# Finishing the preceding step's down tiles first, in a fused two-layer feed-forward kernel

## The chip, the cores and the metric

The kernel runs on one core of a Trainium2 chip. The metric is the device time of one execution in microseconds. TensorE (PE) does the matmuls, ScalarE (ACT) the activations and copies, VectorE (DVE) the elementwise work, SyncE (SP) issues the transfers, GpSimd (POOL) helps at the start.

## The reference

Three stages over 8192 tokens of 192 values, all float32:

```python
x = attn(x, weight_gen)                 # softmax over 7 taps, a causal window of 7 tokens, 8 heads
g = x @ w_gate                          # layer 1, 192 -> 1536
x = (g * sigmoid(g)) * (x @ w_val) @ w_out
h = x @ w_in                            # layer 2, 192 -> 2048
x = (h * clip(h + 3, 0, 6) / 6) @ w_out2
```

## The kernel before, in words

**Blocks and periods.** The tokens are cut into BLOCKS = 16 blocks of 512 columns. Period i (0 to 16) does layer 1 of block i and layer 2 of block i-1. Layer 1 has N1 = 12 tiles of 128 hidden units, layer 2 has N2 = 16; tiles are numbered n = 0 to 11 and N1 + 0 to N1 + 15. Periods 2 to 14 are a loop, the others are written out.

**Precision.** Each float32 operand is split into a rounded high part (hi) and a remainder (lo), and a product is taken as hi x hi, hi x lo (of the weights) and hi x lo (of the data). ACT makes the high parts (L438 for the hidden values), DVE the remainders (L672).

**Tiles.** An up product gives a hidden tile, a down product adds it to the layer's sum. D = 192 = 128 + 64, and the 64 left over (the tail) is packed. On PE everything works on half of the array's rows: LOW is the first 64 partitions, HIGH the last 64, and an instruction in one half can run beside one in the other. An up bank of PSUM is begun by one half and finished by the other; `s_halves` keeps them apart. The sums of a layer are the accumulator pair `acc1` or `acc2`; `s_down_half` separates the halves there.

**Steps.** PE's order is written out by hand. `gated_step` handles one tile of layer 1 (gate and value: 18 half-instructions) and one down product (10). `plain_step` handles two tiles of layer 2 (18) and two down products (20). A down product lags by LAG = 4 tiles, and `hid_hi` and `hid_lo` are rings of RING = 4. In both steps the order is: begin the up banks, begin the down products, finish the up banks, finish the down products. Plain step j handles tiles N1+2j and N1+2j+1 and takes down N1+2j-4 and N1+2j-3.

**Other engines.** Per tile, ACT does `bend` (Silu L429 in layer 1, Relu L431 in layer 2) and then `round_hi` of the tile before; DVE does `tile_product` (L664 or L667), `between(i, n, 0)`, `tile_lo` of the tile before (L672), `between(i, n, 1)`. `bend` of a tile waits for `tile_lo` two tiles back, since there are two hidden buffers; `round_hi` waits until the ring's place is free (`s_down`). `between` hands out the other work one piece at a time: the 18 operations of the next block's convolution (k = 2n + slot), `fold_output` (L704) at n = 10, `input2_lo` (L692) at n = 9, `sum_tail` (L698) at n = N1+3, and `input1_lo` (L679, L686) at n = N1+7 and N1+8. ACT has `take_sum2` at n = 4, `take_rows` at n = N1, `take_sum1` at n = N1+3, `input1_hi` (L450, L453) at n = N1+7.

**Transposes.** `transpose_output(i-2)` (L980, L985) stands between the gated and the plain steps and writes to `acc2`. `transpose_input(i+1)` (L961, L967) stands after plain step j = 3 and writes to `acc1`. Both are twelve small instructions.

**Waits of a down product.** `down_ready` (L813) waits for `s_hid_lo` of its tile and, at the first tile of a layer, for the accumulators to be free: for layer 2 that is `s_out_rows`, the copy of the output rows. `up_ready` waits for `s_hidden`, the products of all tiles up to two steps back.

Of the kernel before, what the change touches and what calls it, by code (L numbers as in the profile page):

```python
# [35 lines left out]
P = 128  # L36
# [3 lines left out]
LAG = 4  # L40
WARM_SLOTS = 66
# [3 lines left out]
def swiglu_hardswish_kernel(nc, x, taps_in, w_gate, w_val, w1_out, w2_in, w2_out, out):  # L45
# [54 lines left out]
    with ExitStack() as ctx:  # L100
# [128 lines left out]
        def input_banks(b):  # L229


            return acc_pair[2 if isinstance(b, int) and b == 1 else 1]
# [46 lines left out]
        def _(sp):  # L279
            def load_piece(q):  # L280
# [6 lines left out]
                elif kind == "tail":  # L287
                    for half in range(2):
                        dst = buf[half * TAIL:(half + 1) * TAIL, 0:CW // y]
                        if y == 1:  # L290
                            src = (w_val, w_gate)[half][P:D, col:col + CW]
                        else:
                            dst = dst.rearrange("r (j c) -> r j c", c=P)
                            src = w[P:D, col:col + CW].rearrange("r (j b c) -> r j b c", b=2, c=P)[:, :, 1 - half, :]
                        sp.dma_start(dst, src).then_inc(s_stage[q % STAGES], 16)
# [106 lines left out]
        def _(act):  # L402
# [44 lines left out]
            def input1_hi(b):  # L447
                banks = input_banks(b)
                act.wait_ge(s_in_cols, b + 1)
                nc.scalar.copy(by_half(inp[1]["hi"][:, :]), main_cols(banks)).then_inc(s_in1_hi, 1)  # L450
                for par in range(2):
                    for half in halves:
                        last = nc.scalar.copy(by_parity_half(inp[1]["tail_hi"][half, :])[:, :, par, :, :],  # L453
                                              tail_cols(banks, halves[par]))
                last.then_inc(s_in1_hi, 1)
# [29 lines left out]
            def period(i):  # L485
# [11 lines left out]
                for n in tiles:  # L497
# [14 lines left out]
                    if n == (N1 + 3 if fixed(i, BLOCKS) else N1) and has_out:  # L512
                        take_rows(i - 2)
                    if n == N1 + 3 and not fixed(i, BLOCKS):
                        take_sum1(i)
                    if n == N1 + 7 and has_next:
                        input1_hi(i + 1)
                if fixed(i, 0):
                    round_hi(i, N1 - 1)
                    input1_hi(1)  # L520
                    take_sum1(0)
# [10 lines left out]
            input1_hi(0)  # L532
            periods(act, period)
# [8 lines left out]
        def _(dve):  # L542
# [132 lines left out]
            def input1_lo(b, part):  # L675
# [6 lines left out]
                for par in range(2):  # L682
                    for half in halves:
                        hi, lo = (by_parity_half(inp[1][name][half, :])[:, :, par, :, :]
                                  for name in ("tail_hi", "tail_lo"))
                        last = nc.vector.tensor_tensor(lo, tail_cols(banks, halves[par]), as_f32(hi), ALU.subtract)  # L686
                last.then_inc(s_in1_lo, 1)
# [21 lines left out]
            def between(i, n, slot):  # L709

                has_next = not (fixed(i, BLOCKS - 1) or fixed(i, BLOCKS))
                k = 2 * n + slot - (HALF + 1 if fixed(i, 0) else 0)
                if k < -HALF:
# [9 lines left out]
                elif n == N1 - 2 and slot == 0 and not (fixed(i, 0) or fixed(i, 1) or fixed(i, BLOCKS)):  # L723
                    fold_output(i - 2)
                elif n == N1 - 3 and not fixed(i, 0):
                    input2_lo(i - 1, slot)
                elif n == N1 + 3 and slot == 1 and not fixed(i, BLOCKS):
                    sum_tail(i)
                elif n in (N1 + 7, N1 + 8) and slot == 1 and has_next:
                    input1_lo(i + 1, n - N1 - 7)  # L730

            def period(i):
# [13 lines left out]
                if fixed(i, 0):  # L746
                    tile_lo(i, N1 - 1)
                    input1_lo(1, 0)
                    input1_lo(1, 1)
                    sum_tail(0)  # L750
# [16 lines left out]
            input1_lo(0, 1)  # L767
            shift_max(rest[PARTS - 2], rest[PARTS - 1])
# [5 lines left out]
        def _(pe):  # L774
# [38 lines left out]
            def down_ready(i, n):  # L813
# [4 lines left out]
                if i == 1 and n == 0:  # L818
                    pe.wait_ge(s_mid, 1)
                if y == 2 and k == 0 and i < BLOCKS:  # L820
                    wait(pe, s_out_rows, i - 1)
# [16 lines left out]
            def operands(at):  # L838
                _, kind, n = steps[at]
                even, odd = up_bank[2 * (n % 2)], up_bank[2 * (n % 2) + 1]  # L840
                if kind == "gated":
                    return 1, (even, n * P), (odd, F1 + n * P), n * P
                return 2, (even, 2 * n * P), (odd, (2 * n + 1) * P), n * P

            def up_halves(at):
                y, (even, even_col), (odd, odd_col), _ = operands(at)
                up_ready(at)
                for product in range(3):
                    up_main(LOW, even, y, even_col, product, first=True)
                    mm = up_main(HIGH, odd, y, odd_col, product, first=True)  # L850
                mm.then_inc(s_halves, 1)

            def up_alone(at):
                up_halves(at)
                up_halves(at + 1)
                for one in (at, at + 1):
                    y, (even, even_col), (odd, odd_col), col = operands(one)
                    pe.wait_ge(s_halves, one + 1)
                    for product in range(3):
                        up_main(HIGH, even, y, even_col, product)  # L860
                        up_main(LOW, odd, y, odd_col, product)
                    for product in range(2):
                        up_tail(HIGH, even, y, col, product)
                        up_tail(LOW, odd, y, col, product)
                    up_tail(HIGH, even, y, col, 2).then_inc(s_first, 1)
                    up_tail(LOW, odd, y, col, 2).then_inc(s_val if y == 1 else s_first, 1)

            def gated_step(i, n, di, d):
                at = number[i, "gated", n]
                y, (gate, gate_col), (val, val_col), col = operands(at)  # L870
                down_steps[0] += 1
                up_halves(at)
                wait(pe, s_down, tile_no(di, d))
                down_ready(di, d)
# [4 lines left out]
                down_main(LOW, d, 2).then_inc(s_down_half, 1)  # L879
                pe.wait_ge(s_halves, at + 1)  # L880
                up_main(HIGH, gate, y, gate_col, 0)
                up_main(LOW, val, y, val_col, 0)
                up_main(HIGH, gate, y, gate_col, 1)
                up_main(LOW, val, y, val_col, 1)
                up_main(HIGH, gate, y, gate_col, 2)
                up_main(LOW, val, y, val_col, 2)
                up_tail(HIGH, gate, y, col, 0)
                up_tail(LOW, val, y, col, 0)
                up_tail(HIGH, gate, y, col, 1)
                up_tail(LOW, val, y, col, 1)  # L890
                up_tail(HIGH, gate, y, col, 2).then_inc(s_first, 1)
                up_tail(LOW, val, y, col, 2).then_inc(s_val, 1)
                pe.wait_ge(s_down_half, down_steps[0])
                down_main(HIGH, d, 0)
                down_tail(LOW, d, 0)
                down_main(HIGH, d, 1)
                down_tail(LOW, d, 1)
                down_main(HIGH, d, 2).then_inc(s_down, 1)

            def plain_step(i, j, c, d):  # L900
                at = number[i, "plain", j]
                y, (even, even_col), (odd, odd_col), col = operands(at)
                down_steps[0] += 1
                up_halves(at)
                wait(pe, s_down, tile_no(i, c))
                down_ready(i, c)
                down_main(LOW, c, 0)
                down_tail(HIGH, c, 0)
                down_main(LOW, c, 1)
                down_tail(HIGH, c, 1)  # L910
                down_main(LOW, c, 2)
                down_ready(i, d)
                down_tail(HIGH, d, 0)
                down_main(LOW, d, 0)
                down_tail(HIGH, d, 1)
                down_main(LOW, d, 1)
                pe.wait_ge(s_halves, at + 1)
                up_main(HIGH, even, y, even_col, 0)
                down_main(LOW, d, 2).then_inc(s_down_half, 1)
                up_main(HIGH, even, y, even_col, 1)  # L920
                up_main(LOW, odd, y, odd_col, 0)
                up_main(HIGH, even, y, even_col, 2)
                up_main(LOW, odd, y, odd_col, 1)
                up_tail(HIGH, even, y, col, 0)
                up_main(LOW, odd, y, odd_col, 2)
                up_tail(HIGH, even, y, col, 1)
                up_tail(LOW, odd, y, col, 0)
                up_tail(HIGH, even, y, col, 2).then_inc(s_first, 1)
                up_tail(LOW, odd, y, col, 1)
                pe.wait_ge(s_down_half, down_steps[0])  # L930
                down_main(HIGH, c, 0)
                up_tail(LOW, odd, y, col, 2).then_inc(s_first, 1)
                down_main(HIGH, c, 1)
                down_tail(LOW, c, 0)
                down_main(HIGH, c, 2)
                down_tail(LOW, c, 1).then_inc(s_down, 1)
                down_main(HIGH, d, 0)
                down_tail(LOW, d, 0)
# [115 lines left out]
```

## Time and profile before

| | us |
|---|---|
| median of 3 runs | 1271.58 (1271.38 to 1272.57) |
| the profiled execution | 1271.35 |
| its span, first to last instruction | 1269.5 |
| PE busy | 1220.7 |
| DVE busy | 881.0 |
| ACT busy | 650.9 |

The profile is of one execution. A timeline row gives the start, the time, the engine and line, the operation, what it writes and reads, and the count of merged instructions; a bracket holds the engine's idle time before it and what ended it. A merged row (x2) covers both instructions from the first's start to the last's end. PE is the matmuls, PEld the weight loads, which overlap them. In the mean PE is busy in 96% of the span, and the chain that ended last runs through it for 70%.

### The profile page before, as it was taken

To read this page: it belongs to the slowest core of one execution; us is meant where nothing else is said; L and a number is where in the kernel's file an instruction comes from. 1 tells how busy PE (TensorE), PEld (TensorE's weight loads), DVE (VectorE), ACT (ScalarE), POOL (GpSimd) and SP (SyncE) were. 2 spreads that over 40 slices of the span, in tenths; PEclk is the share of its full clock that TensorE was granted. 3 is DMA by queue.
4 is the path that set the end of the run, shared out by engine and by line. 5 is a ranking of instruction groups with operands and counts; after the bars stand their busy time and mean duration, and the time that the engine had idled before them with its cause. 6 is when DMAs were issued, how large, how long until landed. Compare 5 with 4: busy or idle time off the path is not lost.

```text
span 1269.5 us, 26488 instructions
## 1 busy us (share of the span) xinstructions
PE 1220.7 (96%) x10696; PEld 1032.1 (81%) x10696; DVE 881.0 (69%) x1353; ACT 650.9 (51%) x1178; POOL 57.6 (5%) x43
## 2 busy tenths in 40 slices
PE   5779999999999999999999999999999999999998
PEld 4557888888898888888888888888889888888876
DVE  7688676676867768686776867667686766864554
ACT  1554654546455453645546464554645545364554
POOL 6441100000000000000000000000000000000000
PEclk9899999999999999999999999999999999999999
DMA  5330001001010100101000010100101010000000
GB/s 163 87 112 23 11 1 44 2 1 44 1 45 1 39 7 1 45 1 44 1 22 24 1 44 2 44 1 7 39 2 44 1 44 2 1 13 1 14 13 14
DMA packets 11766, 32.00 MB, mean 25 GB/s; under 512 B 1048, under 2 KB 5784, under 8 KB 11544
## 3 DMA queue, kind: packets, MB, share of 16 engines
q1 hardware_dynamic: 11672, 30.53, 7.4%
q8 instruction: 85, 1.39, 0.5%
q14 instruction: 9, 0.07, 0.0%
HBM read 24.24 MB, written 6.29 MB: 24 GB/s over the span
## 4 chain that ended last, share of the span: by engine, by line
PE 70%; DVE 13%; ACT 11%; issue 3%; DMA 1%; POOL 0%; ACTq 0%; SPq 0%; POOLq 0%
PE up_bank L787 27%; PE acc L802 16%; PE up_bank L793 14%; PE acc L809 11%; DVE hid_lo L672 6%; DVE hidden L667 5%; ACT hidden L431 5%; DVE in_tail_lo L686 2%; ACT hid_hi L438 1%; PE up_bank L1024 1%; ACT in_tail_hi L453 1%; DMA stage<-in_moe_w_gate_dram 1%; DMA stage<-in_moe_w_val_dram 1%; ACT in_hi L450 1%; ACT swapped L461 1%
## 5 line engine op out<-in xcount | busy, mean ns | idle before, releaser
L787 PE MATMUL up_bank<-in_hi,up_hi 64*128 64x512 f32 x1280 | 350.7, 395 | 18.0 <-DVE hidden L664 12.3
L809 PE MATMUL acc<-hid_hi,dn_tail 64*128 64x512 f32 x872 | 342.4, 393 | 11.6 <-DVE hid_lo L672 10.7
L787 PE MATMUL up_bank<-in_hi,up_lo 64*128 64x512 f32 x1280 | 346.2, 388 | 0.0
L787 PE MATMUL up_bank<-in_lo,up_hi 64*128 64x512 f32 x1280 | 345.9, 388 | 0.0
L802 PE MATMUL acc<-hid_hi,dn_hi 64*128 64x512 f32 x872 | 342.3, 393 | 0.0
L802 PE MATMUL acc<-hid_lo,dn_hi 64*128 64x512 f32 x872 | 337.4, 387 | 0.0
L802 PE MATMUL acc<-hid_hi,dn_lo 64*128 64x512 f32 x872 | 337.3, 387 | 0.0
L809 PE MATMUL acc<-hid_lo,dn_tail 64*128 64x512 f32 x872 | 337.3, 387 | 0.0
L667 DVE SCALAR_TENSOR_TENSOR hidden<-hidden,up_bank 128x512 f32<-128x512 f32 x256 | 176.1, 688 | 209.7 <-ACT hidden L431 208.5
L672 DVE TENSOR_TENSOR hid_lo<-hidden,hid_hi 128x512 fp32r<-128x512 f32 x448 | 313.0, 699 | 1.0
L431 ACT ACTIVATE hidden<-up_bank,half_col 128x512 f32<-128x512 f32 x256 | 176.4, 690 | 242.0 <-DVE hid_lo L672 129.7
L429 ACT ACTIVATE hidden<-up_bank 128x512 f32<-128x512 f32 x192 | 114.9, 598 | 333.2 <-PE up_bank L793 290.8
L438 ACT CAST hid_hi<-hidden 128x512 fp32r<-128x512 f32 x448 | 273.5, 610 | 1.1 <-DVE hidden L667 0.8
L787 PEld LDWEIGHTS up_bank<-in_hi,up_hi 64*128 64x128 f32 x1280 | 198.6, 185 | 44.2 <-DVE hidden L664 18.1
L664 DVE TENSOR_TENSOR hidden<-hidden,up_bank 128x512 f32<-128x512 f32 x192 | 132.0, 687 | 127.3 <-ACT hidden L429 116.0
L787 PEld LDWEIGHTS up_bank<-in_lo,up_hi 64*128 64x128 f32 x1280 | 198.6, 185 | 20.3
L787 PEld LDWEIGHTS up_bank<-in_hi,up_lo 64*128 64x128 f32 x1280 | 198.8, 185 | 19.6
L809 PEld LDWEIGHTS acc<-hid_hi,dn_tail 64*128 64x128 f32 x872 | 160.5, 184 | 41.6 <-DVE hid_lo L672 30.6
L802 PEld LDWEIGHTS acc<-hid_hi,dn_hi 64*128 64x128 f32 x872 | 160.5, 184 | 13.4 <-issue 0.4
L802 PEld LDWEIGHTS acc<-hid_hi,dn_lo 64*128 64x128 f32 x872 | 160.7, 184 | 12.9
L802 PEld LDWEIGHTS acc<-hid_lo,dn_hi 64*128 64x128 f32 x872 | 160.6, 184 | 13.0
L809 PEld LDWEIGHTS acc<-hid_lo,dn_tail 64*128 64x128 f32 x872 | 160.7, 184 | 9.4
(87 smaller groups left out, 1400.1 us busy)
## 6 DMA issues: line engine op xcount, KB each, us to landing
window<-in_x_dram SPq DMA_DIRECT2D x14, 960.0 KB
out_dram<-out_rows SPq DMA_DIRECT2D x16, 384.0 KB, 2.3
stage<-in_moe_w_out_dram SPq DMA_DIRECT2D x7, 384.0 KB, 3.5
window<-in_x_dram SPq DMA_DIRECT2D x4, 472.5 KB
taps<-in_weight_gen_dram SPq DMA_DIRECT2D x1, 1568.0 KB, 13.0
stage<-in_moe_w_in_dram SPq DMA_DIRECT2D x4, 256.0 KB, 2.7
stage<-in_moe_w_gate_dram SPq DMA_DIRECT2D x3, 256.0 KB, 2.7
stage<-in_moe_w_val_dram SPq DMA_DIRECT2D x3, 256.0 KB, 8.3
```

The costliest lines, as they stand in the source:

```text
L429: nc.scalar.activation(buf, up_bank[2 * (n % 2)][:, :], ACT.Silu).then_inc(s_bent, 1)
L431: nc.scalar.activation(buf, up_bank[n % 4][:, :], ACT.Relu, bias=half_col[:, 0:1], scale=1.0 / 6.0).then_inc(s_bent, 1)
L438: nc.scalar.copy(hid_hi[:, n % RING, :], hidden[:, n % 2, :]).then_inc(s_hid_hi, 1)
L450: nc.scalar.copy(by_half(inp[1]["hi"][:, :]), main_cols(banks)).then_inc(s_in1_hi, 1)
L664: nc.vector.tensor_tensor(buf, buf, up_bank[2 * (n % 2) + 1][:, :], ALU.mult).then_inc(s_hidden, 1)
L667: nc.vector.scalar_tensor_tensor(out=buf, in0=buf, scalar=1.0, in1=up_bank[n % 4][:, :], op0=ALU.min, op1=ALU.mult).then_inc(s_hidden, 1)
L672: nc.vector.tensor_tensor(hid_lo[:, n % RING, :], hidden[:, n % 2, :], as_f32(hid_hi[:, n % RING, :]), ALU.subtract).then_inc(s_hid_lo, 1)
L686: last = nc.vector.tensor_tensor(lo, tail_cols(banks, halves[par]), as_f32(hi), ALU.subtract)
L787: return nc.tensor.matmul(dst[:, :], w[lane[half], col:col + P], a[lane[half], :], start=first and product == 0, stop=False)
L793: return nc.tensor.matmul(dst[:, :], w[lane[half], col:col + P], a[lane[half], :], start=False, stop=product == 2)
L802: return nc.tensor.matmul(acc[y][0], w[lane[half], k, :], a[lane[half], n % RING, :], start=half == LOW and product == 0 and k == 0, stop= ...
L809: return nc.tensor.matmul(acc[y][1], dn_tail[y][lane[half], k, :], a[lane[half], n % RING, :], start=half == HIGH and product == 0 and k == 0,
```

## The change

A step now first finishes the down products that the step before began, and begins its own as its last act. In layer 2 the HIGH half runs one instruction ahead: the first up product of step j+1 is issued at the end of step j (`up_first_high`). The steps are written out for each kind of neighbour (`gated_after_plain`, `plain_after_gated`, openings, `finish_downs`). LAG and RING stay at 4, and each product is computed as before.

Moved besides: `transpose_output` to after gated step 7 with `fold_output` at n = 6 (the later convolution operations shift by one place) and `take_rows` at n = 9; `transpose_input` to after gated step 11, now into `acc2` for all blocks but the first; `input1_hi` to n = N1, N1+1 and N1+2 in three pieces; `input1_lo` to n = N1+2, N1+3, N1+4, slot 1, in three pieces; `input2_lo` to n = 10; `take_sum1` to n = N1+4, `sum_tail` to n = N1+5. The first down product of layer 2 now waits for `s_in1_lo` at 2i+4, which is the last piece of `input1_lo(i+1)`; in period 15 it waits for `s_out_rows`.

```diff
         def input_banks(b):
-            return acc_pair[2 if isinstance(b, int) and b == 1 else 1]
+            return acc_pair[1 if isinstance(b, int) and b == 0 else 2]
...
                 k = 2 * n + slot - (HALF + 1 if fixed(i, 0) else 0)
+                if has_out and (n, slot) == (FOLD_AT, 0):
+                    fold_output(i - 2)
+                    return
+                if has_out and n >= FOLD_AT:
+                    k -= 1
...
-                elif n == N1 - 3 and not fixed(i, 0):
+                elif n == N1 - 2 and not fixed(i, 0):
                     input2_lo(i - 1, slot)
-                elif n == N1 + 3 and slot == 1 and not fixed(i, BLOCKS):
+                elif n in (N1 + 2, N1 + 3, N1 + 4) and slot == 1 and has_next:
+                    input1_lo(i + 1, n - N1 - 2)
+                elif n == N1 + 5 and slot == 1 and not fixed(i, BLOCKS):
                     sum_tail(i)
-                elif n in (N1 + 7, N1 + 8) and slot == 1 and has_next:
-                    input1_lo(i + 1, n - N1 - 7)
...
-                if y == 2 and k == 0 and i < BLOCKS:
-                    wait(pe, s_out_rows, i - 1)
+                if y == 2 and k == 0 and i < BLOCKS - 1:
+                    pe.wait_ge(s_in1_lo, 2 * i + 4)
+                elif y == 2 and k == 0 and i == BLOCKS - 1:
+                    pe.wait_ge(s_out_rows, i - 1)
...
+            def gated_step(i, n, p, di, d):
+                at = number[i, "gated", n]
+                up_begin(at)
+                may_finish_downs()
+                down_tail(LOW, p, 0)
+                down_main(HIGH, p, 0)
+                down_tail(LOW, p, 1)
+                down_main(HIGH, p, 1)
+                pe.wait_ge(s_halves, at + 1)
+                low_up(at, 0)
+                down_main(HIGH, p, 2).then_inc(s_down, 1)
+                low_up(at, 1)
+                high_up(at, 0)
...
+                low_up(at, 5)
+                high_up(at, 4)
+                may_begin_down(di, d)
+                down_main(LOW, d, 0)
+                high_up(at, 5)
+                down_main(LOW, d, 1)
+                down_tail(HIGH, d, 0)
+                down_main(LOW, d, 2)
+                down_tail(HIGH, d, 1).then_inc(s_down_half, 1)
...
+            def begin_two_downs(i, j, c, d, last_up):
+                may_begin_down(i, c)
+                down_main(LOW, c, 0)
+                last_up()
+                down_main(LOW, c, 1)
+                down_tail(HIGH, c, 0)
+                down_main(LOW, c, 2)
+                down_tail(HIGH, c, 1)
+                down_ready(i, d)
...
+                down_main(LOW, d, 2).then_inc(s_down_half, 1)
+                if j + 1 < N2 // 2:
+                    up_first_high(number[i, "plain", j + 1])
+                elif i + 1 < BLOCKS:
+                    up_first_high(number[i + 1, "gated", 0])
...
+            def plain_step(i, j, p, q, c, d):
+                at = number[i, "plain", j]
+                up_begin(at, begun=True)
+                may_finish_downs()
+                down_main(HIGH, p, 0)
...
+                low_up(at, 5)
+                high_up(at, 4)
+                begin_two_downs(i, j, c, d, lambda: high_up(at, 5))
...
             def transpose_input(b):
                 pe.wait_ge(s_conv_rows, b + 1)
                 banks = input_banks(b)
-                if b != 1:
-                    wait(pe, s_mid, b)
+                if b > 2:
+                    pe.wait_ge(s_out_rows, b - 2)
...
+                    if n == ROWS_AFTER and i >= 2:
+                        transpose_output(i - 2)
+                if i + 1 < BLOCKS:
+                    transpose_input(i + 1)
+                for j in range(N2 // 2):
+                    c = N1 + 2 * j - LAG
+                    if j == 0:
+                        plain_after_gated(i, c - 1, c, c + 1)
+                    else:
+                        plain_step(i, j, c - 2, c - 1, c, c + 1)
```

## Rows read from the trace of the kernel before

**Rows 1.** The page's head: busy time and share of the span.

```profile
PE 1220.7 (96%) x10696; PEld 1032.1 (81%) x10696; DVE 881.0 (69%) x1353; ACT 650.9 (51%) x1178; POOL 57.6 (5%) x43
```

**Rows 2.** Timeline of PE: start us, us, engine, line, operation; two gated steps.

```profile
620.90 0.61 PE L787 MATMUL up_bank<-in_hi,up_hi 64*128 64x512 f32 x2
621.12 0.61 PE L787 MATMUL up_bank<-in_hi,up_lo 64*128 64x512 f32 x2
...
624.07 0.61 PE L787 MATMUL up_bank<-in_hi,up_hi 64*128 64x512 f32 x2
```

**Rows 3.** Timeline of PE at the output transposes of two periods and an input group.

```profile
655.81 0.44 PE L980 MATMUL acc<-ident,out_main 64*128 64x64 f32 x5
...
674.05 0.44 PE L961 MATMUL acc<-ident,conv_main 64*128 64x64 f32 x5
...
674.74 0.57 PE L787 MATMUL up_bank<-in_hi,up_lo 64*128 64x512 f32 x2
...
731.02 0.28 PE L980 MATMUL acc<-ident,out_main 64*128 64x64 f32 x2
```

**Rows 4.** Waits (total us, times, longest): whole run, then 656 to 731 us.

```profile
PEld acc L809 <- DVE hid_lo L672: 30.6, 45, 1.5
...
PEld acc L809 <- DVE hid_lo L672: 2.0, 3, 0.9
```

**Rows 5.** Timeline around one such wait.

```profile
670.21 0.68 DVE L672 TENSOR_TENSOR hid_lo<-hidden,hid_hi 128x512 fp32r<-128x512 f32 x1
...
670.95 0.49 PE L809 MATMUL acc<-hid_hi,dn_tail 64*128 64x512 f32 x1 [0.21 <-DVE hid_lo L672]
...
671.28 0.39 PE L809 MATMUL acc<-hid_lo,dn_tail 64*128 64x512 f32 x1
```

**Rows 6.** Timelines of ACT and DVE in a calm plain step.

```profile
687.69 0.69 ACT L431 ACTIVATE hidden<-up_bank,half_col 128x512 f32<-128x512 f32 x1 [0.93 <-PE up_bank L793]
...
689.82 0.69 ACT L431 ACTIVATE hidden<-up_bank,half_col 128x512 f32<-128x512 f32 x1 [0.93 <-DVE hid_lo L672]
...
688.41 0.69 DVE L667 SCALAR_TENSOR_TENSOR hidden<-hidden,up_bank 128x512 f32<-128x512 f32 x1 [0.84 <-ACT hidden L431]
689.02 0.68 DVE L672 TENSOR_TENSOR hid_lo<-hidden,hid_hi 128x512 fp32r<-128x512 f32 x1
```

**Rows 7.** Timeline of PE: a matmul that waits for the one before it.

```profile
92.42 0.39 PE L952 MATMUL acc<-hid_lo,dn_tail 128*128 128x512 f32 x1
...
92.86 0.19 PEld L948 LDWEIGHTS acc<-hid_hi,dn_hi 128*128 128x128 f32 x1 [0.48 <-PE acc L952]
...
93.20 0.40 PE L949 MATMUL acc<-hid_hi,dn_lo 128*128 128x512 f32 x1
```

**Rows 8.** Timeline: the last up matmul of a tile, and ACT on its bank.

```profile
651.95 0.39 PE L793 MATMUL up_bank<-in_tail_lo,up_tail_hi 64*128 64x512 f32 x2
...
652.37 0.60 ACT L429 ACTIVATE hidden<-up_bank 128x512 f32<-128x512 f32 x1 [2.07 <-PE up_bank L793]
```

**Rows 9.** Timeline of DVE, 676 to 681 us: the first two tail operations of the split.

```profile
679.68 0.68 DVE L672 TENSOR_TENSOR hid_lo<-hidden,hid_hi 128x512 fp32r<-128x512 f32 x1
680.29 0.84 DVE L686 TENSOR_TENSOR in_tail_lo<-acc,in_tail_hi 64x256 fp32r<-64x256 f32 x2
```

**Rows 10.** PE in stretches (us, busy, count, granted clock, DMA, GB/s), then its timeline.

```profile
51.30:54.10 2.80, 0.01 (x2) 1.00 0.62 178
...
55.30:58.70 3.40, 3.40 (x18) 0.50 0.13 39
...
62.80:64.40 1.60, 0.00 (x0) 1.00 0.71 219
64.50:67.90 3.40, 3.40 (x28) 1.00 0.24 78
...
55.80 1.05 PE L787 MATMUL up_bank<-in_hi,up_lo 64*128 64x512 f32 x2
56.22 1.05 PE L787 MATMUL up_bank<-in_lo,up_hi 64*128 64x512 f32 x2
```

More of the change, by code:

```diff
@@ L681, in input1_lo @@
                     return
[L682 to L687, printed above, removed]
+                par = part - 1
+                for half in halves:
+                    hi, lo = (by_parity_half(inp[1][name][half, :])[:, :, par, :, :]
+                              for name in ("tail_hi", "tail_lo"))
+                    last = nc.vector.tensor_tensor(lo, tail_cols(banks, halves[par]), as_f32(hi), ALU.subtract)
+                if par == 1:
+                    last.then_inc(s_in1_lo, 1)
             def input2_lo(b, part):
@@ L839, in operands @@
                 _, kind, n = steps[at]
-                even, odd = up_bank[2 * (n % 2)], up_bank[2 * (n % 2) + 1]
+                first, second = up_bank[2 * (n % 2)], up_bank[2 * (n % 2) + 1]
                 if kind == "gated":
[L842 to L846, printed above, removed]
-                up_ready(at)
[L848 to L851, printed above, removed]
+                    return 1, (first, n * P), (second, F1 + n * P), n * P
@@ new lines, in operands, with up_begin @@
+                return 2, (second, (2 * n + 1) * P), (first, 2 * n * P), n * P
+            def up_begin(at, begun=False):
+                y, (x, x_col), (z, z_col), _ = operands(at)
+                if not begun:
+                    up_ready(at)
+                    up_main(LOW, x, y, x_col, 0, first=True)
+                    up_main(HIGH, z, y, z_col, 0, first=True)
+                    up_main(LOW, x, y, x_col, 1)
+                    up_main(HIGH, z, y, z_col, 1)
+                    up_main(LOW, x, y, x_col, 2)
+                    up_main(HIGH, z, y, z_col, 2).then_inc(s_halves, 1)
+                else:
+                    up_main(LOW, x, y, x_col, 0, first=True)
+                    up_main(HIGH, z, y, z_col, 1)
+                    up_main(LOW, x, y, x_col, 1)
+                    up_main(HIGH, z, y, z_col, 2)
+                    up_main(LOW, x, y, x_col, 2).then_inc(s_halves, 1)
@@ L853, in up_alone @@
             def up_alone(at):
-                up_halves(at)
-                up_halves(at + 1)
+                up_begin(at)
+                up_begin(at + 1)
                 for one in (at, at + 1):
-                    y, (even, even_col), (odd, odd_col), col = operands(one)
                     pe.wait_ge(s_halves, one + 1)
[L859 to L866, printed above, removed]
@@ L868, in gated_step, with may_finish_downs @@
-            def gated_step(i, n, di, d):
-                at = number[i, "gated", n]
-                y, (gate, gate_col), (val, val_col), col = operands(at)
-                down_steps[0] += 1
-                up_halves(at)
-                wait(pe, s_down, tile_no(di, d))
-                down_ready(di, d)
+                    for k in range(6):
+                        low_up(one, k)
+                        high_up(one, k)
+            def may_finish_downs():
+                pe.wait_ge(s_down_half, down_steps[0])
@@ L943, in down_alone, with finish_downs @@
+            def finish_downs(*tiles):
+                may_finish_downs()
+                for n in tiles:
+                    down_tail(LOW, n, 0)
+                    down_main(HIGH, n, 0)
+                    down_tail(LOW, n, 1)
+                    down_main(HIGH, n, 1)
+                    down_main(HIGH, n, 2).then_inc(s_down, 1)
             def down_alone(i, n):
@@ new lines, in last_period @@
+            def last_period(i):
+                finish_downs(TILES - LAG - 2, TILES - LAG - 1)
+                for n in range(TILES - LAG, TILES):
+                    down_alone(i - 1, n)
+                up_alone(number[i, "plain", 0])
+                transpose_output(i - 2)
+                for j in range(2, N2 // 2):
+                    c = N1 + 2 * j - LAG
+                    if j == 2:
+                        plain_opening(i, j, c, c + 1)
+                    else:
+                        plain_step(i, j, c - 2, c - 1, c, c + 1)
+                finish_downs(TILES - LAG - 2, TILES - LAG - 1)
+                for n in range(TILES - LAG, TILES):
+                    down_alone(i, n)
@@ L1027, in _ @@
             transpose_input(0)
-            for i in range(BLOCKS + 1):
+            first_period()
+            for i in range(1, BLOCKS):
                 period(i)
+            last_period(BLOCKS)
             transpose_output(BLOCKS - 1)
```

271 lines of the change are left out of this document (173 added, 98 removed).

## The prediction

> **What bounds the kernel now.** First the page's head: PE is busy 1220.7 of 1269.5 us, DVE 881.0, ACT about half of it [rows 1]. So TensorE is the bound, but a busy engine says nothing of whether it could go faster; for that I read its timeline. An instruction here works on one half of the array's rows (lane LOW or HIGH), and two run side by side. In both lanes starts follow each other at 0.2266 us; I call this a slot. A gated step has 28 half-instructions, 14 slots, and one step starts 3.17 us after the last, which is 14 x 0.2266 [rows 2]. So a gated step has no hole at all. A plain step (two tiles, 38 halves) would be 19 slots, 4.31 us.
>
> Next I ask what a period costs over its slots. 12 gated and 8 plain steps are 12 x 14 + 8 x 19 = 320 slots, 72.50 us. The output transposes of two neighbouring periods start at 655.81 and 731.02, 75.21 apart [rows 3]. 2.71 us are over. The group of the input starts at 674.05 and the second up product behind it at 674.74, where without transposes it would be 0.23 behind [rows 3]: 0.46 us, and as much for the output group, 0.92 together. The remaining 1.79 us per period are waits, and the list of waits names them: weight loads of the down product at L809 for DVE's hid_lo, 45 in the run, 3 in this period, 1.5 us at most [rows 4]. One of them shows their shape: LOW and HIGH stop, the load starts with its matmul at 670.95, 0.06 us after hid_lo ends at 670.89, and the matmul behind it comes 0.33 us after the first instead of 0.23, so a restart costs 0.11 more [rows 5]. They all lie in layer 2, in the steps where DVE and ACT have extra work (the sum of layer 1, the split of the next input). Periods 1 to 14 hold 42 of them and period 15 has 2; at 1.6 to 1.8 us a period and 0.9 in the last I put them at 25.2 us in all. The 45th, in period 16, is about 1.4 us.
>
> **The down product begun last.** Nothing is added: a gated step is still 28 halves, a plain one 38, in strict alternation of the lanes. The first down product of a plain step starts in slot 14 instead of 4, its second in slot 17 instead of about 6, so hid_lo may come about 10 slots, 2.4 us, later. The largest wait seen is 1.5 us [rows 4]. All 45 waits fall within that margin: -25.2 -1.4 = -26.6 us. What is late next? The up bank of step j+1 is asked for at the end of step j and needs the product of the second tile of step j-1. From a calm step: first Relu 0, its product +0.72, hid_lo +1.33, next first Relu +4.31, a step later [rows 6]; the second Relu of a step comes at +2.13 and its product ends at +3.54, and PE asks at about +5.0. So 1.4 us are spare. The ring of four is tighter: hid_hi of a step's first tile now has to wait for a down product that finishes in slot 5 of the next step. That step starts at -0.42 - 12 slots + 4.31 = +1.17, its slot 5 at +2.08, seen 0.42 later at +2.5; ACT is there at +2.7. 0.2 us spare, no cost.
>
> Waits inside PE: what a later matmul may see of an earlier one is 0.44 us from start to weight load, with 0.11 more to the matmul [rows 7], 0.55 in all. The new gated step asks for its halves 3 slots (0.68 us) after they start, 0.57 at least where the lanes stand half a slot apart. The weight load normally starts one slot ahead of the matmul, at 0.45. I cost it at nothing; from both sides it is 0 to 0.1 us in some 170 gated steps.
>
> **Transposes and the input work moved.** The two transpose groups stay at 0.46 us. The output group now follows gated step 7 and needs DVE's fold, put at tile 6 in place of one convolution step; the fold takes 0.84 us like its neighbours, and step 7 ends 1 us later than that. The convolution ends at tile 9, the input group comes after tile 11: spare. SP's window load hangs on the convolution and its store on the rows copied out at tile 9 instead of 12: neither is later, and no DMA is added. ACT's and DVE's pieces of the input split, one per tile, fit in the time in which each waits for the other [rows 6].
>
> But the input transposes now land in the second accumulator pair, where layer 2 sums. So down_ready has a new wait: the first down product of layer 2 waits until the whole of input i+1 is split (s_in1_lo at 2i+4). That product is tile c of plain step j=2 (c = N1+2j-4). And the last piece of the split is given out by DVE at n = N1+4, slot 1: behind the product of tile N1+4 and hid_lo of N1+3. Tile N1+4 is the first tile of this same step j=2, whose up product ends just before. PE can't be served before DVE has gone through that tile. The chain, from the start of the last up matmul of N1+4:
> - PE to ACT 0.42 (matmul 651.95, Silu 652.37) [rows 8]
> - Relu to DVE's product 0.72, product to hid_lo 0.61 [rows 6]
> - hid_lo to the tail split 0.61, two of its 64x256 operations 0.84 [rows 9]
> - end on DVE to weight load 0.06 [rows 5]
>
> Sum 3.26. Without the wait the matmul would start 0.23 after that up matmul; with it 0.11 after the late load. Hole: 3.26 + 0.11 - 0.23 = 3.14 us. No slack elsewhere shortens it, since the producer's input comes from PE itself two instructions earlier. Behind the waiting load in PE's queue stand the last up product of the second tile, both down products and the next step's first up; ACT waits for the first of these. ACT and DVE have caught up by then, so the later steps are calm. Condition: has_next, i = 1 to 14. 14 x 3.14 = +44.0 us. Period 15 waits for out_rows there, long done.
>
> **Edges.** Six places wait at once for what has just been issued (the two openings of the down products, the plain opening, three times finish_downs): 0.44 + 0.11 - 0.23 = 0.32 each [rows 7], and three unpaired slots of 0.23: 2.6 us. Those of the first period stand beside ACT and DVE, which set its pace. I take +2.0; bounds 0 and 2.6.
>
> **The clock.** 1271.6 - 26.6 + 44.0 + 2.0 = 1291 would be all if TensorE kept its clock. In each hole it stands idle for 2.9 us (3.26 less the 0.39 of the matmul running). The trace has a hole of 2.8 us in the first period, and 1.2 us behind its end the granted clock is 0.50 (1.2 GHz) for 3.4 us, starts 0.42 us apart instead of 0.23; behind a hole of 1.6 us it stays 1.00 (2.4 GHz) [rows 10]. At half clock 3.4 us hold 8 slots instead of 15: 7 x 0.2266 = 1.6 us lost. The new hole is of the larger kind. The fall in the trace came with a delay, so where a hole lies decides whether it comes; I take 10 of 14, +16 us, with 0 and 14 (+22) as bounds. Sum: 1307.
>
> The Trainium skill has a rule here (page "TensorE: Matmul & The Clock Gate", section on HAM oscillation in real kernels): where every round of a loop has a wait long enough to re-throttle, the transition is paid in every round and not once. By that rule all 14 would pay, which gives 1291 + 22 = 1313; the trace agrees as far as one hole of 2.8 us can show it.
>
> **Rivals.**
> 1. The hole as computed, the clock holds in most of them: 1291 (1286 to 1297). For it: two holes of 1.6 cost no clock, and one event is thin evidence. Against: 2.9 is above the 2.8 that did.
> 2. More waits than one: the halves in gated steps are asked for too early. It decides once lanes stand more than half a slot apart, as they do behind the transposes. 0.1 us in each of 170 steps is +17: about 1324. Against: a late lane corrects itself, because only the leading lane waits.
> 3. Faster: the new wait is met in time and only the gain is left, 1271.6 - 26.6 + 2.0 = 1247. This decides if the split of the input ends 3.2 us earlier than DVE's order has it, one tile pair. Against it stands the order written out in between(), which I followed tile by tile; for it, only an error of mine in that.
> That the change doesn't do what it says would be that the old waits stay as well: 1307 + 26.6. For that hid_lo would have to come 2.4 us later than it was wanted, and the longest wait is 1.5 [rows 4]; its chance is within rival 2's.
>
> **How the numbers follow.** The sum is made against the profiled execution, 1271.35 us (span 1269.5), which is 0.2 from the median of 1271.58. Forecast 1307 with chance 0.68, own range 1298 to 1316; rival 1 0.19; rival 2 0.08; rival 3 0.05. Range 1286 to 1318: it leaves out rival 3, most of rival 2 and the thin ends. 0.2% is 2.5 us, about what a measurement of this kernel tells from no change. Slower: the first three, 0.94; faster 0.05; 0.01 for a meeting in the middle.
>
> **What would show it.** In the profile after: no PE wait for hid_lo at L809 in layer 2; instead one wait per period for in_tail_lo, 14 in all, each near 3.1 us, PE's largest; the distance of output transposes about 76.6 us, or some 78 where the clock fell; a granted clock below 1.00 in stretches of 3.4 us behind the holes, mean about 0.98. Wrong would be: no such wait, a second family of waits, or a clock row that stays 1.00.

## The result and the profile after

The changed kernel takes 1317.47 us (1316.96 to 1317.64, 4 runs), the one before 1272.07 us (1271.38 to 1272.98). The ratio is 1.0356 with a 95% interval of 1.0338 to 1.0374: 3.6% slower. The forecast was 1307 us with a range of 1286 to 1318.

The head of the profile after, to be read against [rows 1]: the same number of matmuls, a span longer by 46 us, and PE busy for a smaller share of it.

```profile
span 1315.7 us, 26501 instructions
PE 1233.1 (94%) x10696; PEld 1076.9 (82%) x10696; DVE 880.4 (67%) x1353; ACT 652.6 (50%) x1178; POOL 57.1 (4%) x43
```

PE's list of waits after (total us, times, longest). The line that answers to [rows 4], for hid_lo, is gone; the first line is new.

```profile
PE acc L821 <- DVE in_tail_lo L698: 43.3, 14, 3.1
PE up_bank L806 <- DVE hidden L676: 13.8, 10, 2.7
PE up_bank L1203 <- ACT up_hi L410: 12.2, 1, 12.2
PE up_bank L806 <- DVE in_tail_lo L698: 4.4, 1, 4.4
```

14 waits of up to 3.1 us, one in each of periods 1 to 14. The other three lines are the start and the first two periods, as in the kernel before. The timeline of one such wait, ACT, DVE and PE sorted by start, with lines left out:

```profile
612.65 0.39 PE L812 MATMUL up_bank<-in_tail_lo,up_tail_hi 64*128 64x512 f32 x1
...
613.07 0.69 ACT L433 ACTIVATE hidden<-up_bank,half_col 128x512 f32<-128x512 f32 x1 [1.06 <-PE up_bank L812]
...
613.79 0.69 DVE L679 SCALAR_TENSOR_TENSOR hidden<-hidden,up_bank 128x512 f32<-128x512 f32 x1 [0.21 <-ACT hidden L433]
...
614.40 0.69 DVE L684 TENSOR_TENSOR hid_lo<-hidden,hid_hi 128x512 fp32r<-128x512 f32 x1
...
615.12 0.87 DVE L698 TENSOR_TENSOR in_tail_lo<-acc,in_tail_hi 64x256 fp32r<-64x256 f32 x2
...
616.13 0.48 PE L821 MATMUL acc<-hid_hi,dn_hi 64*128 64x512 f32 x1 [3.09 <-DVE in_tail_lo L698]
616.13 0.54 PE L812 MATMUL up_bank<-in_tail_lo,up_tail_hi 64*128 64x512 f32 x1
```

It is the chain of the forecast, link by link: the last up matmul of tile N1+4, its Relu, its product, hid_lo of the tile before, the last piece of the input's split, and only then the first down product of layer 2. From 612.65 to 616.13 are 3.48 us. The last row shows what is queued behind the wait: the last up product of the second tile.

PE in stretches around it (stretch, us, busy, count, granted clock, DMA share, GB/s):

```profile
591.00:613.00 22.00, 22.00 (x204) 1.00 0.18 63
613.10:616.10 3.00, 0.00 (x0) 1.00 0.00 0
616.40:619.80 3.40, 3.40 (x18) 0.51 0.02 5
619.90:666.00 46.10, 46.10 (x410) 1.00 0.00 1
```

Behind the hole the granted clock is 0.51, that is 1.2 GHz, for 3.4 us. The trace shows such a stretch at the end of every one of the 14 holes; it begins 0.1 us before the end of the first and 0.7 us behind the end of the last. The mean clock of the run is 0.978 instead of 0.996. The rows that answer to [rows 3], the output transposes of two neighbouring periods:

```profile
588.16 0.40 PE L1136 MATMUL acc<-ident,out_main 64*128 64x64 f32 x8
...
666.61 0.41 PE L1136 MATMUL acc<-ident,out_main 64*128 64x64 f32 x8
```

78.45 us lie between them, 75.21 before. 3.24 more in 14 periods are 45.4 us, which is the whole loss.

### The profile page after: what moved, and what is told of

Same layout as the page of the kernel before. It is cut to its first block, busy times and chain, and to the rows that moved or that the text cites. A ratio compares the mean times of both kernels' runs of the same rounds, so it can differ in the third digit from the quotient of the medians.

```text
span 1315.7 us, 26501 instructions
## 1 busy us (share of the span) xinstructions
PE 1233.1 (94%) x10696; PEld 1076.9 (82%) x10696; DVE 880.4 (67%) x1353; ACT 652.6 (50%) x1178; POOL 57.1 (4%) x43
## 4 chain that ended last, share of the span: by engine, by line
PE 89%; DVE 6%; ACT 2%; DMA 1%; issue 1%; POOL 0%; SPq 0%; ACTq 0%; DVEq 0%; POOLq 0%
PE up_bank L806 33%; PE acc L821 23%; PE up_bank L812 16%; PE acc L828 15%; DVE hid_lo L684 1%; DVE in_tail_lo L698 1%; ACT hidden L433 1%; DVE hidden L679 1%; DMA window<-in_x_dram 1%; DMA stage<-in_moe_w_val_dram 1%; DVE prod_even L571 1%; PE acc L1104 0%; DVE prod_odd L571 0%; PE acc L1117 0%; DVE sum_even L575 0%
## 5 line engine op out<-in xcount | busy, mean ns | idle before, releaser
L806 PE MATMUL up_bank<-in_hi,up_hi 64*128 64x512 f32 x1280 | 360.6, 400 | 19.4 <-DVE hidden L676 13.8
L806 PE MATMUL up_bank<-in_hi,up_lo 64*128 64x512 f32 x1280 | 355.3, 393 | 0.0
L806 PE MATMUL up_bank<-in_lo,up_hi 64*128 64x512 f32 x1280 | 354.3, 392 | 0.0
L828 PE MATMUL acc<-hid_lo,dn_tail 64*128 64x512 f32 x872 | 343.7, 394 | 0.0
L821 PE MATMUL acc<-hid_lo,dn_hi 64*128 64x512 f32 x872 | 343.5, 394 | 0.0
L821 PE MATMUL acc<-hid_hi,dn_lo 64*128 64x512 f32 x872 | 343.3, 394 | 0.0
L806 PEld LDWEIGHTS up_bank<-in_hi,up_hi 64*128 64x128 f32 x1280 | 203.1, 188 | 44.0 <-DVE hidden L676 19.7
L812 PE MATMUL up_bank<-in_tail_lo,up_tail_hi 64*128 64x512 f32 x640 | 203.7, 391 | 0.0
L812 PE MATMUL up_bank<-in_tail_hi,up_tail_hi 64*128 64x512 f32 x640 | 199.0, 387 | 0.0
L812 PE MATMUL up_bank<-in_tail_hi,up_tail_lo 64*128 64x512 f32 x640 | 198.8, 387 | 0.0
```

The source lines that it names most:

```text
L806: return nc.tensor.matmul(dst[:, :], w[lane[half], col:col + P], a[lane[half], :], start=first and product == 0, stop=False)
L812: return nc.tensor.matmul(dst[:, :], w[lane[half], col:col + P], a[lane[half], :], start=False, stop=product == 2)
L821: return nc.tensor.matmul(acc[y][0], w[lane[half], k, :], a[lane[half], n % RING, :], start=half == LOW and product == 0 and k == 0, stop= ...
L828: return nc.tensor.matmul(acc[y][1], dn_tail[y][lane[half], k, :], a[lane[half], n % RING, :], start=half == HIGH and product == 0 and k == 0,
```

## The experiments

The rivals were: (A) the wait for the input's split and the clock behind it are the whole loss; (B) the new order of the steps costs something itself; (C) the clock falls, or not, for another reason. All times are medians. A ratio is to the kernel before, run on the same chip.

**The input work put back (e1_input_later).** All else of the change stays.

```diff
-            return acc_pair[1 if isinstance(b, int) and b == 0 else 2]
+            return acc_pair[2 if isinstance(b, int) and b == 1 else 1]
-                    if n == N1 and has_next:
+                    if n == N1 + 7 and has_next:
                         input1_hi(i + 1)
-                elif n in (N1 + 2, N1 + 3, N1 + 4) and slot == 1 and has_next:
-                    input1_lo(i + 1, n - N1 - 2)
+                elif n in (N1 + 9, N1 + 10, N1 + 11) and slot == 1 and has_next:
+                    input1_lo(i + 1, n - N1 - 9)
-                if y == 2 and k == 0 and i < BLOCKS - 1:
-                    pe.wait_ge(s_in1_lo, 2 * i + 4)
...
+                if y == 2 and k == 0 and i < BLOCKS:
+                    wait(pe, s_out_rows, i - 1)
...
+                    if j == 3 and i + 1 < BLOCKS:
+                        transpose_input(i + 1)
```

> The changed kernel with one part undone: the input transposes stand after plain step 3 again and write to acc1, ACT's pieces of the split come at tiles N1+7 to N1+9 and DVE's at N1+9 to N1+11, and the first down product of layer 2 waits for the copied output rows as in the kernel before. The new order of the down products, the upper half ahead and the moved output work stay. Theory (all of the loss is the wait for the input split and the clock behind it, 3.4 + 1.65 us a period): no wait of PE in layer 2, granted clock 1.00 after the start, 1317.5 - 14 x 5.05 = 1247 us. Rival (the new order of the steps costs something by itself): above 1260 us, with PE waits in gated steps or inside PE. Rival that the old waits for hid_lo stay: about 1272 us.

Measured: 1251.01 us against 1271.81, ratio 0.9836 (0.9819 to 0.9852). The 14 waits are gone, no wait for hid_lo has come in their place, and the clock stays at 1.00 after the first period. So the new order costs nothing that shows here; B falls. 4 us are missing to the 1247 expected: the periods last 73.73 us, 0.28 more than in the next run. The timeline of PE's weight loads shows them idle ahead of the input transposes, for nothing that the profile names:

```profile
590.35 0.36 PEld L1115 LDWEIGHTS acc<-ident,conv_main 64*128 64x128 f32 x8 [0.35 <-issue]
```

There the transposes stand between an up product already begun in one half and the rest of it; whether that is the reason is asked below.

**The split given out two tiles earlier (e4_two_earlier).** The wait stays in PE's program.

```diff
-                    if n == N1 and has_next:
+                    if n == N1 - 1 and has_next and not fixed(i, 0):
                         input1_hi(i + 1)
-                    if n in (N1 + 1, N1 + 2) and has_next:
-                        input1_tail_hi(i + 1, n - N1 - 1)
+                    if n in (N1 - 1, N1) and has_next and not fixed(i, 0):
+                        input1_tail_hi(i + 1, n - N1 + 1)
-                elif n in (N1 + 2, N1 + 3, N1 + 4) and slot == 1 and has_next:
-                    input1_lo(i + 1, n - N1 - 2)
+                elif n in (N1, N1 + 1, N1 + 2) and slot == 1 and has_next:
+                    input1_lo(i + 1, n - N1)
-                if i + 1 < BLOCKS:
-                    transpose_input(i + 1)
...
+                    if n == N1 - 2 and i + 1 < BLOCKS:
+                        transpose_input(i + 1)
```

> The changed kernel with the input transposes after gated step 10 instead of 11, and every piece of the input split on ACT and DVE given out earlier, so that DVE's last piece is at tile N1+2 instead of N1+4. The wait on PE stays, in the same place. Theory: the last piece ends about 1 us before PE asks, no hole, clock 1.00, 1317.5 - 14 x 5.05 = 1247 us, like the kernel with the input work put back. Rival (it isn't the time of the last piece but the sharing of acc2 or the wait itself that costs): stays above 1290 us.

Measured: 1247.07 us, ratio 0.9803 (0.9787 to 0.982). It beats both kernels by changing only when the pieces are given out, and with them the input transposes, one gated step earlier. The output transposes of two periods:

```profile
558.47 0.35 PE L1136 MATMUL acc<-ident,out_main 64*128 64x64 f32 x6
...
631.92 0.29 PE L1136 MATMUL acc<-ident,out_main 64*128 64x64 f32 x4
```

73.45 us, that is 72.50 of slots and 0.95 for the two groups of transposes: no hole is left in a period. Neither the sharing of acc2 nor the wait as such costs anything.

**One tile earlier (e3_one_earlier).** As above, by one tile: DVE's pieces at N1+1 to N1+3, and the input transposes stay after gated step 11.

```diff
-                    if n in (N1 + 1, N1 + 2) and has_next:
-                        input1_tail_hi(i + 1, n - N1 - 1)
+                    if n in (N1, N1 + 1) and has_next:
+                        input1_tail_hi(i + 1, n - N1)
-                elif n in (N1 + 2, N1 + 3, N1 + 4) and slot == 1 and has_next:
-                    input1_lo(i + 1, n - N1 - 2)
+                elif n in (N1 + 1, N1 + 2, N1 + 3) and slot == 1 and has_next:
+                    input1_lo(i + 1, n - N1 - 1)
```

> The changed kernel with ACT's and DVE's pieces of the input split one tile earlier, DVE's last at N1+3. Theory: the piece no longer depends on the first tile of step 2; from the Relu of tile N1+2 it ends at +4.9 us, PE asks at +3.9, so a hole of about 1.2 us instead of 3.4 stays, 14 times. A hole of that size is below the one of 1.6 us behind which the clock stayed in the kernel before, so the clock stays at 1.00: 1317.5 - 14 x (3.4 - 1.2 + 1.65) = 1264 us. Rival (any hole brings the clock down): 1264 + 23 = 1287 us. Rival (the hole isn't set by DVE's order): 1317 us.

Measured: 1265.77 us, ratio 0.9953 (0.9937 to 0.997). The list of waits has the same line with a third of the time, and the clock stays at 1.00:

```profile
PE acc L821 <- DVE in_tail_lo L698: 14.0, 14, 1.0
```

The three places of the last piece in DVE's order give a series: N1+4 is 3.6% slower than before, N1+3 0.5% faster, N1+2 2.0% faster.

**The hole filled (e2_fill).** The pairs compute nothing that is used. Their number, FILLS, is 12.

```diff
+                if j == 2 and i < BLOCKS - 1:
+                    fill(number[i, "plain", j + 1])
                 may_begin_down(i, c)
```

> The changed kernel with 12 pairs of matmuls put ahead of the wait in plain step 2; their results go to the up banks of the next step, which it overwrites. 12 x 0.2266 = 2.7 us of otherwise empty work in a hole of 3.1 us idle. Theory: the hole stays as long as it was, since DVE sets its end, but the granted clock stays at 1.00, which gives back 14 x 1.65 = 23 us: 1294 us. Rival (the clock falls for something else in that step): it falls 14 times as before and the time is 1317 us. Rival (the filling delays the chain): above 1317 us.

Measured: 1295.17 us, ratio 1.0185 (1.0168 to 1.0202). PE's idle time in the hole is down to 0.4 us (list of waits), and the clock stays (stretch behind it, columns as above):

```profile
PE acc L822 <- DVE in_tail_lo L699: 5.3, 14, 0.4
```

```profile
613.00:680.00 67.00, 67.00 (x610) 1.00 0.06 22
```

The distance to the changed kernel is 22.3 us, 1.59 per hole: the price of the clock, separated from that of the hole.

**Half filled (e8_fill4, e10_fill6).** The same with 4 and with 6 pairs.

> The changed kernel with 4 pairs of empty matmuls ahead of the wait instead of 12, so that TensorE is idle for about 2.2 us in each hole, between the 1.7 us that kept the clock and the 2.75 us that didn't. The hole ends where it did. If each such hole costs the clock: 1317 us. If none does: 1294 us, as with 12 pairs. My reading in the prediction (the place of the hole decides): some pay and some don't, 1300 to 1312 us, and stretches of 0.50 in the clock rows behind only part of the 14 holes.

Measured with 4 pairs: 1316.42 us, ratio 1.0352 (1.0331 to 1.0372). 13 of 14 holes cost the clock. The first hole and the second:

```profile
142.30:144.50 2.20, 0.00 (x0) 1.00 0.00 0
144.60:148.00 3.40, 3.40 (x30) 1.00 0.00 0
219.20:221.30 2.10, 0.00 (x0) 1.00 0.00 0
222.00:225.40 3.40, 3.40 (x20) 0.50 0.00 0
```

Both are 2.2 us; the first is followed by 30 matmuls in 3.4 us, the second by 20 in the same time at half clock.

> The changed kernel with 6 pairs of empty matmuls ahead of the wait, idle time in the hole about 1.75 us. With 4 pairs and 2.2 us idle, 13 of 14 holes cost the clock; the holes of 1.6 and 1.77 us in the first period of several runs cost nothing. If size alone decides: the clock stays 1.00, 1294 us. If the place of the hole decides too: some pay, 1297 to 1312 us. If it doesn't matter how long TensorE is idle but only that it waits: 1317 us.

Measured with 6 pairs: 1294.57 us, ratio 1.0186 (1.0157 to 1.0216); no hole costs the clock, with up to 1.8 us idle:

```profile
PE acc L822 <- DVE in_tail_lo L699: 24.3, 14, 1.8
```

So at this place up to 1.8 us cost nothing in 14 of 14 holes, 2.2 us the clock in 13 of 14, 3.1 us in 14 of 14. That size decides alone is not shown: the holes of one run lie alike, and the first period, where PE waits for DVE's products, shows the contrary. In the run with the input work put back it has a hole of 3.17 us behind which the clock stays at 1.00; in the 1247 us run the hole at the same place, 3.10 us, has the clock at 0.50 from 53.5 to 60.3:

```profile
54.29 0.50 PE L806 MATMUL up_bank<-in_hi,up_hi 64*128 64x512 f32 x2 [3.17 <-DVE hidden L676]
51.20:54.20 3.00, 0.00 (x0) 1.00 0.69 181
54.30:57.70 3.40, 3.40 (x28) 1.00 0.15 39
```

```profile
51.60:54.50 2.90, 0.00 (x0) 0.82 0.75 190
54.60:60.20 5.60, 5.60 (x26) 0.50 0.09 24
```

The first three rows (one of the timeline, then two stretches) are of e1_input_later, the other two of e4_two_earlier.

**A longer hole (e5_longer).** DVE's sum of the layer 1 tail is put ahead of the last piece.

```diff
                 elif n in (N1 + 2, N1 + 3, N1 + 4) and slot == 1 and has_next:
+                    if n == N1 + 4:
+                        sum_tail(i)
                     input1_lo(i + 1, n - N1 - 2)
```

> The changed kernel with DVE's sum of layer 1's tail ahead of the last piece of the input split, both at tile N1+4. The sum waits for ACT's copies, which end 2.9 us behind the Relu of that tile, so the last piece ends at about +4.4 instead of +2.9. Theory (DVE's order sets the end of the hole): PE's idle time in it 4.5 instead of 3.1 us, 14 x 1.45 = 20 us more, 1338 us, with the clock falling once behind each hole for 3.4 us. Rival (the chain is bounded by something else, PE's own restart say): 1317 us. Rival (a longer hole costs the clock for longer): up to 1361 us.

Measured: 1345.42 us, ratio 1.058 (1.0559 to 1.0601), 7 us over the expectation. PE's idle time is 4.7 us in each hole, as computed to 0.2; so DVE's order sets the end. The rest is clock: at 8 of the 14 holes it is low for 6.8 us instead of 3.4, which lies between the theory and the rival of a longer loss. One of the 8, and one of the 6:

```profile
543.70:548.30 4.60, 0.00 (x0) 0.93 0.00 0
548.40:551.00 2.60, 2.60 (x12) 0.50 0.00 0
551.00:554.40 3.40, 3.40 (x18) 0.50 0.00 0
```

```profile
625.00:629.60 4.60, 0.00 (x0) 1.00 0.00 0
629.70:633.00 3.30, 3.30 (x16) 0.50 0.02 5
633.00:636.40 3.40, 3.40 (x32) 1.00 0.00 0
```

All 14 holes are 4.7 us long, so the two kinds don't differ in size. In the 8 the clock falls 0.7 to 1.8 us before PE starts again, in the 6 at most 0.6 us before.

**The moves without the new order (e6_old_order).** The steps of the kernel before, with the moves of the 1247 us run.

```diff
             def plain_step(i, j, c, d):
                 at = number[i, "plain", j]
...
                 up_halves(at)
                 wait(pe, s_down, tile_no(i, c))
                 down_ready(i, c)
                 down_main(LOW, c, 0)
...
+                        if n == N1 - 2 and 0 < i < BLOCKS - 1:
+                            transpose_input(i + 1)
```

> The moves alone: transposes, fold, copied rows and input work as in the run with DVE's last piece at tile N1+2 (1247 us), but PE's steps in the order of the kernel before (own down products in the middle of the step, no upper half ahead; the layer 2 tail weights in their old halves). Theory (the new order buys about 2.4 us of margin for hid_lo, the old one has next to none): the first down product of layer 2 is asked for at slot 4 of step 2, 1.3 us before the split of the input is done, a hole of about 1.3 us; the wait for hid_lo behind the sum of layer 1 stays at about 0.6, and some small ones: 72.5 + 0.9 + 1.3 + 0.6 + 0.3 = 75.6 us a period, about 1277 us, clock 1.00. Rival (the margin comes from giving the input work out in small pieces earlier, and the order of the down products doesn't matter): about 1250 us.

Measured: 1275.74 us, ratio 1.0031 (1.0018 to 1.0043). PE waits for both things:

```profile
PEld acc L828 <- DVE hid_lo L684: 10.4, 17, 1.5
...
PE acc L821 <- DVE in_tail_lo L698: 14.9, 14, 1.1
```

With the same moves the new order is worth 1275.74 - 1247.07 = 28.7 us. Of the old 45 waits for hid_lo 17 are left in spite of the old order, so a part of them came from where the extra work stood. With the new order neither wait is left. The rival (the order doesn't matter) falls.

**No upper half ahead (e7_no_slot_ahead).** On the 1247 us run.

```diff
-                if j + 1 < N2 // 2:
-                    up_first_high(number[i, "plain", j + 1])
-                elif i + 1 < BLOCKS:
-                    up_first_high(number[i + 1, "gated", 0])
```

> The run with DVE's last piece at tile N1+2 (1247 us), but without the upper half ahead in layer 2: the first upper up product is issued in its own step again. Theory (a plain step is 38 halves in two lanes of 19 either way, and no wait inside PE comes nearer than 3 slots): 1247 us within 2 us, periods of 73.45 us. Rival (the slot ahead hides a latency between the halves): 0.1 to 0.3 us more in each of some 120 plain steps, 1259 us or more.

Measured: 1246.93 us, ratio 0.9804 (0.9788 to 0.982), the same as with it. This part of the change is worth nothing here.

**No upper half ahead, input work put back (e11_later_not_ahead).** The same edit on the first experiment's kernel (1251.01 us), to see whether its 0.28 us a period go.

> The run with the input work put back (1251.0 us, periods of 73.73 us), but without the upper half ahead in layer 2. Theory (the 0.24 us a period too much there come from the input transposes standing between an up product already begun in one half and the rest of it): periods of 73.45 us, 1247.5 us, and no weight loads at the up product with idle time named issue, 14 times. Rival (they come from the place of the transposes or of the split as such): 1251 us, unchanged.

Measured: 1254.62 us, ratio 0.9872 (0.9856 to 0.9889): neither. The periods are 73.96 us, and the weight loads of the input transposes sit idle for up to 0.5 us once per period:

```profile
PEld acc L1111 <- issue: 5.9, 14, 0.5
```

So the theory falls: without an up product begun ahead the idle time is longer, not gone. Both traces have the reason, though the list calls it "issue". At this place `transpose_input` also waits for `s_mid`, DVE's sum of layer 1's tail, and the change moved that sum from tile N1+3 to N1+5. From e1_input_later, with lines left out:

```profile
589.56 0.68 DVE L711 TENSOR_TENSOR mid_tail<-swapped,acc 128x512 f32<-128x512 f32 x1
...
590.35 0.26 PEld L1115 LDWEIGHTS acc<-ident,conv_main 64*128 64x128 f32 x5 [0.35 <-issue]
```

The sum ends at 590.24, and the first weight load starts 0.12 us behind it, as in all 14 periods of both runs. In the kernel before, the sum ends 4.2 us ahead of these transposes, in the same place, and they don't wait. In the 1247 us run they wait for other semaphores. No run moves the sum back, so this rests on the traces. It accounts for the 0.28 us a period that the first experiment lacked; with the half ahead PE has one instruction more to do before the wait, and loses 0.2 us less.

## Why the prediction was right, and where it was short

1. *The old waits go, -26.6 us.* Right. The 1247.07 us of the run without a hole, against 1271.81, are -24.7; with the +2.0 for the edges the forecast had -24.6. The two terms are confirmed as a sum; the periods alone went from 75.21 to 73.45 us, and the forecast had 1.79 of waits in each.
2. *No other wait comes up.* Right for PE: in periods 2 to 14 of the changed kernel it has nothing but the new wait, though the halves in the gated steps are asked for 3 slots after they start. Rival 2 is out. The ring, put at 0.2 us to spare, was short behind the hole: there ACT's rounding waits for a down product once a period. Without the hole this wait is gone too, and PE never waits for what it delays.

```profile
ACT hid_hi L440 <- PE acc L821: 43.1, 14, 3.2
```

3. *The new wait, 14 holes of 3.14 us.* Right in place, count and links; the size was 3.36 (3.48 + 0.11 - 0.23). The links that were short: hid_lo to the tail split 0.72 instead of 0.61, the two operations 0.87 instead of 0.84, their end to the matmul 0.14 instead of 0.06. The row in [rows 9] was of the first two tail operations; those in the chain are the last two. Both read the upper 64 partitions of the bank; the first writes the lower ones, the second the upper. In the 1247 us run, where nothing of ACT's copies lies beside them, the two kinds stand next to each other:

```profile
578.22 0.68 DVE L684 TENSOR_TENSOR hid_lo<-hidden,hid_hi 128x512 fp32r<-128x512 f32 x1
578.82 0.84 DVE L698 TENSOR_TENSOR in_tail_lo<-acc,in_tail_hi 64x256 fp32r<-64x256 f32 x2
...
580.40 0.68 DVE L684 TENSOR_TENSOR hid_lo<-hidden,hid_hi 128x512 fp32r<-128x512 f32 x1
581.12 0.87 DVE L698 TENSOR_TENSOR in_tail_lo<-acc,in_tail_hi 64x256 fp32r<-64x256 f32 x2
```

0.60 and 0.72 us apart. Why is not shown. The crossing from upper to lower alone doesn't cost it: in the kernel before the four operations follow each other, and the last two end 0.88 us behind the first two (1.72 less the 0.84 of [rows 9]), with no such gap between them.

```profile
680.29 1.72 DVE L686 TENSOR_TENSOR in_tail_lo<-acc,in_tail_hi 64x256 fp32r<-64x256 f32 x4
```

The whole term: 14 x 0.22 = 3.1 us short.

4. *The clock, 10 of 14 at 1.6 us.* The price was right (1.59), the count wasn't: 14 of 14. The step that failed was to count the 14 holes as if some would lie well and some badly, from one fall in [rows 10] that came 1.2 us late. They lie alike, 78.4 us apart, and all paid; even at 2.2 us 13 of 14 did. That place matters at all is borne out (a hole of 3.17 us in a first period cost nothing), but how it does is open, and 10 had no more behind it than 14. The rule of the Trainium skill (page "TensorE: Matmul & The Clock Gate", HAM oscillation in real kernels), that a loop in which every round waits long enough to bring the clock down pays the transition every round, gave 1313, and the trace agrees with 14 of 14. +6.3 us.
5. *The edges, +2.0 us.* Not measured alone; right to 0.1 in the sum with the first term.

The idle time of the hole was put at 2.9 us and is 3.1, from the longer chain. 1307 + 3.1 + 6.3 = 1316.4, against 1317.5; 1.1 us are not attributed.

## What to carry to other kernels

When a buffer is shared anew, find the instruction that frees it and ask what stands ahead of it in its engine's queue; here the freeing piece was queued behind work whose input the waiting engine itself had only just issued, which no margin elsewhere could cover. The cure was to give out the same pieces two tiles earlier. Where the profile names no releaser, look in the program for the semaphore: the idle time that ended 0.12 us behind DVE's sum was such a wait. And price a hole on TensorE twice: for its length, and for the clock behind it.

## What the runs showed of the hardware

- In layer 2, one hole per period of up to 1.8 us in TensorE's work left the granted clock alone in 14 of 14 cases, one of 2.2 us brought it to 0.50 for 3.4 us in 13 of 14, one of 3.1 us in 14 of 14, and one of 4.7 us for 6.8 us in 8 of 14 and 3.4 us in the other 6. In the first period a hole of 3.17 us left it alone and one of 3.10 us brought it down. Size is not all, and what else decides is open.
- Each fall of 3.4 us behind the holes of 3.1 us cost 1.6 us. Empty matmuls in these holes, which did not shorten them, gave back 22.3 of 45 us.
- A weight load that waited for a DVE operation of 128x512 started 0.12 us behind its end in 28 of 28 cases, and the profile called the wait "issue".
- Behind an operation of 128x512, the first of DVE's last two tail operations started 0.72 us after its start, the first of the first two 0.60; cause open.
